# Dynamic convolution and two-layer MLP on one core: the second tile moved to the array's halves, and three reorderings in the first six tiles

## The reference

```
w = softmax(weight_gen, axis=-1)                 # (4, 4096, 8 heads, 7 taps)
y[b, s, head h] = sum_k w[b, s, h, k] * x_padded[b, s + k, head h]   # 7 rows, the own one and the six before
h = y @ w_in                                      # (16384, 192) @ (192, 2048)
g = max(0.01 * h, h)
out = g @ w_out                                   # (16384, 2048) @ (2048, 192)
```

## Time and profile before

| | us |
|---|---|
| three runs: median (lowest to highest) | 1036.52 (1036.15 to 1036.73) |
| profiled execution: device time | 1037.43 |
| profiled execution: span from first to last instruction | 1035.6 |
| PE busy, share of the span | 1022.9, 99% |
| DVE busy | 947.1, 91% |
| ACT busy | 631.2, 61% |
| POOL busy | 548.9, 53% |

### The profile page before, as it was taken

One profiled execution on the slowest core, in us unless ns is written; L12 is line 12 of the kernel. 1 busy time (PEld: TensorE's weight loads), 2 busy tenths in 40 slices (PEclk: granted clock), 3 DMA queues, 4 the chain that ended last, 5 costly groups with the idle time before them and its releaser, 6 DMA issues.

```text
span 1035.6 us, 28951 instructions
## 1 busy us (share of the span) xinstructions
PE 1022.9 (99%) x12755; PEld 673.8 (65%) x12755; DVE 947.1 (91%) x1226; ACT 631.2 (61%) x1332; POOL 548.9 (53%) x369
## 2 busy tenths in 40 slices
PE   8999999999999999999999999999999999999998
PEld 3566556566666666666666666666666666666667
DVE  7999999999999999999999999999999999998611
ACT  6766566565565665565665565665566565566554
POOL 0004556475665565565565566566556556556543
PEclk9999999999999999999999999999999999999999
DMA  9101213112131210313111131210313102121100
GB/s 265 64 16 32 82 35 97 34 33 74 26 97 35 81 48 5 97 35 97 35 32 66 35 97 34 57 65 11 97 34 97 34 20 79 34 35 35 34 17 17
DMA packets 67445, 57.48 MB, mean 55 GB/s; under 512 B 56252, under 2 KB 60604, under 8 KB 65336
## 3 DMA queue, kind: packets, MB, share of 16 engines
q1 hardware_dynamic: 67196, 55.35, 19.4%
q10 hardware_dynamic: 124, 0.29, 0.1%
HBM read 29.34 MB, written 12.58 MB: 40 GB/s over the span
## 4 chain that ended last, share of the span: by engine, by line
PE 82%; DVE 16%; ACT 1%; DMA 0%; issue 0%; ACTq 0%; DVEq 0%
PE h_ps L957 40%; PE t_ps L1067 21%; PE out_ps L1067 20%; DVE conv L611 4%; DVE prod L604 4%; DVE gl L653 3%; PE h_ps L1105 1%; DVE conv L604 1%; DVE x_top L616 1%; DVE xs L641 1%; DMA xbuf<-in_x_dram 0%; DVE x_unscale L583 0%; DVE xs L643 0%; DVE wo L633 0%; ACT xs L410 0%
## 5 line engine op out<-in xcount | busy, mean ns | idle before, releaser
L297 POOL TENSOR_TENSOR gl<-g,gh 128x512 f16<-128x512 f32 x360 | 546.9, 1546 | 478.3 <-ACT g L425 478.3
L423 ACT ACTIVATE gh<-h_ps 128x512 f16<-128x512 f32 x512 | 317.2, 620 | 370.2 <-PE h_ps L957 357.8
L1067 PE MATMUL t_ps<-wo,gh 64*128 64x384 f16 (+1 forms) x1984 | 387.8, 318 | 2.4 <-ACT gh L423 2.4
L1067 PE MATMUL out_ps<-wo,gh 64*128 64x384 f16 (+1 forms) x1984 | 387.8, 318 | 0.0
L957 PE MATMUL h_ps<-xT,whA 64*128 64x512 f16 x1920 | 378.3, 376 | 0.0
L425 ACT ACTIVATE g<-h_ps 128x512 f32<-128x512 f32 x512 | 321.7, 628 | 0.0
L611 DVE TENSOR_TENSOR conv<-conv,prod 128x768 f32<-128x768 f32 x186 | 279.6, 1503 | 1.1
L604 DVE TENSOR_TENSOR prod<-xbuf,taps 128x768 f32<-128x768 f32 x186 | 275.7, 1495 | 0.0
L1067 PE MATMUL t_ps<-wo,gl 64*128 64x192 f16 x1920 | 233.5, 243 | 0.0
L1067 PE MATMUL out_ps<-wo,gl 64*128 64x192 f16 x1920 | 233.5, 243 | 0.0
L1067 PEld LDWEIGHTS t_ps<-wo,gh 64*128 64x128 f16 x1984 | 181.6, 94 | 49.1 <-ACT gh L423 2.9
(11 more groups left out here) (99 smaller groups left out, 677.7 us busy)
## 6 DMA issues: line engine op xcount, KB each, us to landing
xbuf<-in_x_dram SPq DMA_DIRECT2D x15, 1344.0 KB, 6.0
out_dram<-stage SPq DMA_DIRECT2D x31, 384.0 KB, 2.3
taps<-in_weight_gen_dram SPq DMA_DIRECT2D x16, 224.0 KB, 6.1
xT_again<-xT SPq DMA_DIRECT2D x29, 64.0 KB, 2.2
rawO<-in_moe_w_out_dram SPq DMA_DIRECT2D x4, 384.0 KB, 9.7
rawA<-in_moe_w_in_dram SPq DMA_DIRECT2D x2, 512.0 KB, 7.9
xbuf<-in_x_dram SPq DMA_DIRECT2D x2, 384.0 KB, 6.5
rawD<-in_moe_w_in_dram SPq DMA_DIRECT2D x1, 512.0 KB, 6.2
```

Source lines behind the costliest of these rows:

```text
L297: nc.gpsimd.tensor_tensor(gl[:, f % RING, :], g[:, f % RING, :], gh[:, f % RING, :], ALU.subtract).then_inc(s_gl_p, 1)
L423: nc.scalar.activation(gh[:, f % RING, :], h_ps[f % GROUP][:], ACT.Prelu, scale=SHRINK, alpha=SLOPE).then_inc(s_gh, 1)
L1067: ins = nc.tensor.matmul(dst, a[rows, f % RING, j * P:(j + 1) * P], moved, start=i == 0 and k < 2 and a is gh and f == 0 and part != 1, st ...
```

## The change

The change has four parts, none of which alters what is computed.

1. **Tile 1 on the halves.** `HALF_FROM = 1` takes over from `BY_PE` in all that decides between whole array and halves: groups 5 to 7 use `hidden`, groups 4 to 7 use `project`. Group 4's `hidden_by_pe` stays. Tile 1's output rows lie in four banks, it makes all products with `gh` before those with `gl` (`TURNS_LATE`), and its first product waits until all four rows of tile 0 are copied out.
2. **Tile 2's lo of x ahead of lo of g.** In `second_tile`, `lo_of_x(2)` stands before `group(NG + 2)` and no longer behind it.
3. **Own rows first in tile 0.** The own rows' DMA counts on a semaphore of its own, `s_x_own`. DVE finishes the softmax of the first four positions alone, multiplies what needs only own rows (one whole product, three quarters of a second), waits for the neighbours' rows, makes the rest, and does the other four positions' softmax behind the last addition.
4. **The hi made in tile 5 one group later.** ACT makes hi of tile 6 in the second group of tile 5, and no longer in the first.

```diff
+        HALF_FROM = 1
...
-            return TURNS_LATE if n // NG == 2 or n == N_GROUPS - 1 else TURNS_WHOLE
+            return TURNS_LATE if n // NG <= 2 or n == N_GROUPS - 1 else TURNS_WHOLE
...
-            sp.dma_start(xbuf[:, 0, HALO * D:(HALO + SUB) * D], x_rows[:, 0:SUB * D]).then_inc(s_x0, DMA)
+            sp.dma_start(xbuf[:, 0, HALO * D:(HALO + SUB) * D], x_rows[:, 0:SUB * D]).then_inc(s_x_own, DMA)
...
-                if i == (1 if m in LATE_TILES else 0) and m + 1 < TILES:
+                if i == (1 if m in LATE_TILES or m - 1 in LATE_TILES else 0) and m + 1 < TILES:
...
+                lo_of_x(2)
                 group(NG + 2)
-                lo_of_x(2)
...
-            for ops in (range(0, 2), range(2, N_SOFTMAX)):
-                for half in range(2):
-                    for n in ops:
-                        softmax0(half, n)
+            for half in range(2):
+                for n in range(2):
+                    softmax0(half, n)
+            for n in range(2, N_SOFTMAX):
+                softmax0(0, n)
             dve.wait_ge(s_softmax0[0], N_SOFTMAX)
-            dve.wait_ge(s_x0, (1 + 2 * B) * DMA)
-            for k in range(K):
-                product0(k)
-
-            dve.wait_ge(s_prod0, K)
+
+            dve.wait_ge(s_x_own, DMA)
+            product0(0)
+            product0(1, 1, SUB)
+            dve.wait_ge(s_x0, 2 * B * DMA)
+            product0(1, 0, 1)
+            for n in range(2, K):
+                product0(n)
+
+            dve.wait_ge(s_prod0, K + 1)
             nc.vector.tensor_tensor(prods0[5], prods0[5], prods0[6], ALU.add).then_inc(s_prod0, 1)
+
+            for n in range(2, N_SOFTMAX):
+                softmax0(1, n)
...
-                if i == 0:
+                if i == 0 and m >= BY_PE:
                     pe.wait_ge(s_xT, DMA * (m + 1 - BY_PE))
...
-                    if i == 0 and m == BY_PE and k == 0:
+                    if i == 0 and m == HALF_FROM and k == 0:
...
-                elif n + 1 < BY_PE * NG:
+                elif n + 1 < NG:
                     hidden_early(n + 1)
...
-                if n < BY_PE * NG:
+                if n < HALF_FROM * NG:
                     project_early(n)
...
-                    pe.wait_ge(s_prod0, k + 1 if k < K - 2 else K + 1)
+                    pe.wait_ge(s_prod0, 1 if k == 0 else k + 2 if k < K - 2 else K + 2)
```

More of the change, by code:

```diff
@@ L130, in dynconv_mlp @@
         s_taps0 = sem("s_taps0")
+        s_x_own = sem("s_x_own")
         s_x0 = sem("s_x0")
@@ L212, in turns_of @@
         def turns_of(n):
-            return TURNS_LATE if n // NG == 2 or n == N_GROUPS - 1 else TURNS_WHOLE
+            return TURNS_LATE if n // NG <= 2 or n == N_GROUPS - 1 else TURNS_WHOLE
         turns_to = [0]
         for n in range(N_GROUPS):
-            turns_to.append(turns_to[-1] + (len(turns_of(n)) if n >= BY_PE * NG else 0))
+            turns_to.append(turns_to[-1] + (len(turns_of(n)) if n >= HALF_FROM * NG else 0))
         def xT_block(par, b):
@@ L263, in rows_of @@
         def rows_of(m):
-            return range(SUB) if m < BY_PE else ROW_ORDER
+            return range(SUB) if m < HALF_FROM else ROW_ORDER
         def wait_row(engine, m, j):
-            if m < BY_PE:
+            if m < HALF_FROM:
                 engine.wait_ge(s_out_ps, 2 * m + j // 2 + 1)
@@ L757, in w_scales, with product0 @@
                 scale_of_unscale(w_scale[:, n:n + 1], w_unscale[:, n:n + 1]).then_inc(s_w_scale, 1)
-            def product0(k):
-                rows = xbuf[:, 0, k * D:k * D + SUB * D].rearrange("p (r g) -> p r g", g=G)
-                w = taps[:, 0, :].rearrange("p (r k) -> p r k", k=K)[:, 0:SUB * H, k:k + 1]
-                nc.vector.tensor_tensor(prods0[k].rearrange("p (r g) -> p r g", g=G), rows,
-                                        w.to_broadcast([P, SUB * H, G]), ALU.mult).then_inc(s_prod0, 1)
+            def product0(n, first=0, last=SUB):
+                k = K - 1 - n
+                rows = xbuf[:, 0, (k + first) * D:(k + last) * D].rearrange("p (r g) -> p r g", g=G)
+                w = taps[:, 0, :].rearrange("p (r k) -> p r k", k=K)[:, first * H:last * H, k:k + 1]
+                nc.vector.tensor_tensor(prods0[n][:, first * D:last * D].rearrange("p (r g) -> p r g", g=G), rows,
+                                        w.to_broadcast([P, (last - first) * H, G]), ALU.mult).then_inc(s_prod0, 1)
             def scales0():
@@ L980, in hidden @@
                 for pair in (f, f + 2):
-                    pe.wait_ge(s_half, (n - BY_PE * NG) * GROUP + pair - f + 2)
+                    pe.wait_ge(s_half, (n - HALF_FROM * NG - 1) * GROUP + pair - f + 2)
                     for what in SECOND:
@@ L1016, in project_early @@
                     for j in range(SUB):
-                        if f == 0 and m > 0 and j % 2 == 0:
-                            pe.wait_ge(s_out_free, SUB * (m - 1) + j + 2)
                         for part in range(2):
```

2 lines of the change are left out of this document (1 added, 1 removed).

## The result

The changed kernel takes **1039.08 us** (median of 15 executions, 1037.43 to 1042.10), the kernel before beside it 1036.11 (15 executions, 1035.64 to 1037.92). The ratio is 1.0028 with a 95% interval of 1.0021 to 1.0035: 3.0 us slower, above my 1036.4, with the median at the end of the range and seven of the fifteen executions beyond it. What also changed is the spread, 4.7 us against 2.3. The profiled execution took 1037.55 us (span 1035.8) and is among its fastest, while the one of before (1037.43) was among the slowest of its kernel. So the two profiles nearly agree in length although the kernels differ by 3 us, which is the first thing that had to be explained.

A forecast was written before the change was run, and what follows sets the result against it. DVE's late sums(4) was taken to set the time up to 195 us, PE from there. Terms -1.1 + 0.35 - 0.96 + 0.6 + 0.96, rounded -0.1, on 1037.43, less 0.91, gave 1036.4 us; 8-in-10 range 1032.8 to 1039.2.

The forecast's parts named there:

- Start (part 3): Tile 0: own rows' products first let hi of tile 0 and all engines start 1.1 us earlier.
- Part 2: Tile 2: lo of x standing first must wait for ACT's first row, +0.35 us on DVE.
- Earlier groups: Tiles 2 and 3: shifted POOL and DVE overlaps cost +0.6 us, bounds -0.96 to +0.96.
- Group 17: POOL's three lo of g, behind sums(3), hit one DVE scale instruction fewer: -0.96 us.
- Group 21: Ahead of sums(4): POOL's lo of g hit DVE's softmax piece or lo of g once, +0.96 us (0 to +2.9).
- used up there by a new wait below 1 us: Tile 4: PE's lead over DVE would end in a short new wait for sums(3), at no price.
- that rival: POOL's group 21 starts ahead of x_scale; three hits cost 2.9 us, clock perhaps low longer: 1038.3 to 1040.0, say 1039.2; chance 0.18.
- The sum: All terms up to sums(4), whose second row PE awaits in tile 5: -0.15, rounded to -0.1 us.
- I keep the clock's 1.7 us as it was: Behind PE's wait ahead of project(20): idle grows from 2.4 to 3 us, clock loss unchanged (bounds 0 and twice that).
- The wait costs more than it lasts: At project(20): 4.2 us lost, 2.4 idle and the rest slow clock; all returns if PE hardly idles.
- the median = profiled -0.91: Whole kernel: the median of runs lay 0.91 us below the profiled 1037.43, so the forecast subtracts that too.

The follow-up runs named there:

- after_again: The changed kernel profiled once more with no edit: 1039.29 us in one execution, kernel before beside it 1037.37.
- p2_p3: Kernel before with parts 2 and 3 only, tile 1 on the whole array: 1036.55 us, kernel before beside it 1037.37.
- only_p3_b: Second run of the kernel before with part 3 alone: 1036.28 us, kernel before beside it 1037.45.
- the fills: Changed kernel with 19, 14 or 5 matmuls on zeros added ahead of the last half product of hidden(21): 1036.10, 1036.68, 1038.17 us.
- fill14: Changed kernel with 14 matmuls on zeros added in hidden(21): 1036.68 us, kernel before beside it 1037.55.
- fill_before: Kernel before with 11 matmuls on zeros added in hidden(21): 1036.02 us, kernel before beside it 1035.77.
- only_p3: Kernel before with part 3 alone, first run: 1034.55 us, kernel before beside it 1035.85.
- only_p4: Kernel before with part 4 alone: 1036.01 us, kernel before beside it 1035.85.
- before_again: The kernel before profiled once more with no edit: 1036.96 us in one execution, its median beside it 1037.37.
- no_p4_b: Second run of the changed kernel without part 4 (parts 1 to 3): 1035.83 us, kernel before beside it 1037.45.
- p1_p3: Kernel before with parts 1 and 3 only: 1035.52 us, kernel before beside it 1037.37; second run 1035.29, beside 1037.45.
- p1_p3_p4: Changed kernel without part 2: 1035.53 us, kernel before beside it 1037.45.
- no_p4: Changed kernel without part 4 (parts 1 to 3), first run: 1035.78 us, kernel before beside it 1035.77.

## Why the prediction was wrong, step by step

Against the profile that I had, the terms for `sums(4)` came out so, each read from `x_scale` to `x_scale` in the two traces:

- **Start (part 3):** -1.22 (I had -1.1; DVE's lo of tile 0 at 17.93 for 19.15). Right in mechanism and size, in an execution whose weights land at 10.5. What I missed is the next limit just behind: when they land at 11.5 (after_again), ACT's sums of |w| set the start to within 0.2 us, and the gain is 0.05. Part of this is scatter, as the same lo starts between 18.77 and 19.48 in the four profiles with the old start.
- **Part 2:** +0.24 on DVE (I had +0.35), read as p2_p3's stretch over only_p3_b's, 56.47 - 56.23.
- **Earlier groups:** -0.1 where I took +0.6, if the profile of before is the measure (stretch 56.37 less 56.23 less the 0.24). Against its executions with the short stretch (54.55) it is +1.6, beyond my bound of one hit.
- **Group 17:** between -0.7 and -0.9 (I had -0.96). `x_scale` is no longer hit (0.17 at 163.16).
- **Group 21:** +1.93, two hits where I took one. One thing that I had wrong is that PE's lead is "used up there by a new wait below 1 us" in tile 4: there was no such wait, because DVE's `sums(3)` had come 1.53 us earlier too. So PE kept 1.78 us of lead, POOL started at 191.20, and PE idled 4.3 us and not 3. The other is the count: by the earlier trace rows the softmax piece starts 0.73 us and the lo of g 1.27 us behind `x_scale`, so three POOL instructions that start 0.7 to 1.1 us behind it, as in my own numbers, reach both. POOL's 191.20 is ahead of the 191.6 that I had named as the point from which the lock decides, but that rival's mechanism, POOL ahead of `x_scale`, did not come: I had put DVE's lead at 0.8, it was 1.83, and POOL started 0.68 us behind `x_scale`. The rival's 1039.2 is close to what was measured by luck: it has three hits where there were two, and it starts from a profile that already had the fallen clock and the long stretch.

The sum is +0.1 (I had -0.1), and `sums(4)` stands at 195.05. That it came out is partly luck: +1.93 for +0.96 in group 21 was made good by -0.1 for +0.6 in the earlier groups. The forecast of the trace held against that one profile; that of the time did not, and the steps that failed are **two that stand behind the sum**.

The first is "I keep the clock's 1.7 us as it was". The profiled executions both have it, but their kernels do not pay it alike. Behind an idle of 0.85 to 1.14 us it was never seen in a profile (seven), behind 2.3 to 2.4 us in two of six, behind 2.8 and more in all three; the fills give 1036.1, 1036.7, 1038.2 and 1039.1 as a series. (Between executions it varies: four of fill14's eleven have a mean clock of 0.998, and where the clock fell in them is not seen, as they were not profiled.) The longer idle, which my own text says (3 us for 2.4), was priced at nothing. And the 1.7 us were no price in the kernel before: beside its upper level, executions with a mean clock of 0.998 and of 1.00 take the same 1037.1 to 1037.8 in the main. "The wait costs more than it lasts", with 4.2 us to come back, is wrong for that kernel; it is right for the changed one.

The second is "the median = profiled -0.91". I took a constant from an execution that ran 1.3 us above the median of the later 15, instead of asking what made it slow. It had the long stretch and the fallen clock; the profiles taken beside the lower level (fill_before, only_p3, only_p4) have 54.55 us, full clock and, without zeros, an idle of 0.89, and the 1036.11 belongs to that level. (No execution of the unedited kernel with the short stretch was profiled.) From that base the sum reads: start -1.2 (or -0.05), stretch +1.8, tiles 4 to 6 -0.9, group 21 +1.9, clock +1.7 (or +2.3), less the wait of 1.3 for block 7's lo that follows when PE resumes early (at 204.91 in before_again, at 202.82 in only_p3): +2.0 with early weights, +3.8 with late ones, and 3.0 measured. That these add up is an account from single profiles, not a measurement of each term; by the mean clocks of all executions the clock's part may be nearer 3.

The Trainium skill bears on the hits and on the clock. The Trainium skill, SBUF — State Buffer, section "Who interferes with whom", calls the port pair an exclusive lock, and a lock fits what the runs show on either side (DVE's 0.94 to 1.93, POOL's 1.1 to 11.4); that it is not some other way of taking turns is argued and not shown; `sums`, which by that section is exempt, took 0.40 in the changed kernel right under POOL's lo of g (191.20 to 195.41), so here the trace agrees. The Trainium skill, TensorE: Matmul & The Clock Gate, section "HAM oscillation — how this bites in real kernels", says that a wait for data between pieces of work lets the clock be throttled again, so that the next piece starts cold; the traces agree, with the 0.50 behind 2.8 to 4.3 us of idle in all three profiles and behind 2.3 to 2.4 us in two of six.

**Which version is best.** Parts 1 and 3 without 2 and 4 (p1_p3): 0.9985 (0.9977 to 0.9994) and 0.9981 (0.9972 to 0.9990) of the kernel before beside it, both times where that one was at its upper level, and at 1035.3 to 1035.5 still about 0.4 below its lower level, beside which it was not run. It beats both kernels, by 0.15 to 0.2% of the one before, and moved by 0.2 us between its two sets of runs. Part 3 alone is faster at best (1034.55) but has the two levels.

What stays open: what tips the tie at 122.5 us for a whole set of runs, whether part 2 would lengthen the stretch without part 1 where the kernel before has the short one, and whether part 4 alone would cost its hits where that kernel has the long one.

## What to carry to other kernels

Before a profile is taken as the base of a sum, ask whether its own time is typical, and if it lies above the median, look for a hit or a fallen clock in it that the usual execution does not have; a term kept "as it was" is a term too. A lead that one engine gains moves every conflict between two others behind it: here, with parts 1 and 3 in place, parts 2 and 4 cost 3 us only together. Where an engine must wait for one that is late, how long it stands still has a price of its own, and moving one piece out of the way of the wait only helps if the next user of the same late engine has slack.

## What was not expected of the hardware

- One POOL subtraction of 128x512 took 11.39 us while DVE ran products back to back at 0.95, against 1.13 (3.39 for three) in p1_p3_p4, where DVE was mostly in `sums` or waiting.
- A difference of 0.01 to 0.02 us in how POOL's start stands to a DVE addition (0.04 against 0.03 or 0.02 ahead) goes with 1.93 or 0.94 us for that addition, in three profiles each.
- Zeros fed to PE during a wait of 4.3 us made the kernel 3 us faster (1036.10 for 1039.08) although the row that PE waits for came no earlier; the mean clock was 1.00 in eight of eleven executions, and never above 0.998 without the zeros.
- A clock of 0.50 for 3 us behind an idle of 2.3 to 2.4 us cost 0.2 us (first profile against before_again, no_p4_b against no_p4, less their starts), as PE at full clock waited 1.3 us for the lo of block 7.
- The first rows of `moe_w_in` were ready for ACT at 9.94 to 11.54 us in different executions, at nearly the same program start.
